# A small addition moved from ScalarE to VectorE, and GpSimd's work per pair of heads in another order

## The chip, the core and the metric

The kernel runs on one core of a Trainium2 chip. TensorE (PE, whose weight loads are listed as PEld), VectorE (DVE), ScalarE (ACT), GpSimd (POOL) and SyncE (SP) each take their own queue of instructions in order. They meet only at semaphores that the program sets and waits for. The metric is the device time of the whole program in microseconds, lower is better. Before the change it is 1112.01 us, the median of 3 runs (1111.71 to 1112.99).

## What is computed

The program chains three parts: attention with rotary position embedding, a mixture of experts, and a dense layer. Only the attention part is touched. Cut to what matters:

```python
def rotate(x):
    x1, x2 = (x[..., :half], x[..., half:])
    return np.concatenate([x1 * cos - x2 * sin, x1 * sin + x2 * cos], axis=-1)
q_rot, k_rot = (rotate(q), rotate(k))          # q, k, v: 4 x 8 heads, 576 positions, 64 wide
scores = scale * np.matmul(q_rot, k_rot.transpose(0, 1, 3, 2))
scores = scores - np.max(scores, axis=-1, keepdims=True)
attn = np.exp(scores)
attn = attn / (np.sum(attn, axis=-1, keepdims=True) + 1e-09)
x = np.matmul(attn, v)                         # then the experts, then the dense layer
```

The `+ 1e-09` on the row sums is the small addition of the title.

## The kernel before

Attention works on 16 pairs of heads. A pair has 9 tiles of scores (`TILES`), numbered 0 to 8: four of 128 rows for head A, one mixed tile with the last 64 rows of both heads (`MIX`, number 4), four for head B. What feeds a product is kept in two halves: a value rounded to fp32r (`hi`) and what is left of it (`lo`).

**PE** runs one `body` per pair, p. In each of its 9 steps it makes a tile of scores of pair p+1 (L376, or L381 and L385 for the mixed tile), turns a tile of probabilities of pair p by transposes against the identity (L423, L419 for the mixed tile, L415 for its corner), and multiplies turned tiles with v (L444, L447, L450). The turned tiles are called A0, X, A1, A2, C, A3, M, B0 to B3. Step 5 turns M (the mixed rows) and multiplies A3. Step 6 makes scores, turns B0, and multiplies M: this product, `MA`, begins with L444, and its first instruction waits until the `lo` half of M is there. The last product of a pair, `MB`, comes in step 1 of the next body.

**ACT** takes the exponential of each tile (L520), rounds each turned tile to `pt_hi` (L541, L535 for X, L538 for C), and moves the sums out of PSUM (L559, L560). In step 3 its `guard` (L551) adds 1e-9, held in a tile `tiny` of one column, to the 9 row sums of pair p: `guarded`.

**DVE** takes the negated maximum of each tile (L620), and `pt_lo` as what `pt_hi` left (L636). In step 5, between the maximum of tile 5 and `pt_lo` of M, `invert` takes the reciprocal of `guarded` (L641). `normalise` (L652, L654, L660) uses it in the next body.

**POOL** prepares pairs ahead. For pair k, `multiply` forms `by_cos` (L338) and `by_sin` (L339) from `raw`. `add_up` forms `rotated` (L323), `hi` (L326) and `lo` (L332). `split_v` splits v of an earlier pair (L312, L317). The order in the loop is multiply(k), split_v(k-2), add_up(k). `split_v(k)` waits for v to have landed, and until PE has done product MB of pair k-2, since it writes over that pair's tile. `add_up(k)` waits for the transfers that read the last `hi`, and its L332 until the scores of pair k-2 are made.

**SP** issues the transfers. Its `body(p)` waits for L332 of pair p+2, and issues 12 copies of `hi` and `lo` into `k_hh`, `k_ll` and `q_st` (the stacks that the scores read). Then it waits for `split_v(p+1)`, loads v of pair p+2 (5 transfers), stores a tail, waits for `multiply(p+3)` and loads `raw` of pair p+4.

Of the kernel before, what the change touches and what calls it, by code (L numbers as in the profile page):

```python
# [11 lines left out]
ALU = mybir.AluOpType  # L12
ACT = mybir.ActivationFunctionType
AX = mybir.AxisListType

P = 128
# [26 lines left out]
def attention(nc, qk, v, cos, sin, ident, fold, emb_t, route_consts, x_all, lg_all, tail_dram,  # L43
# [7 lines left out]
    with ExitStack() as ctx:  # L51
        def sb(name, shape, dt=F32):
            return ctx.enter_context(nc.sbuf_tensor(name, shape, dt))

        def sem(name):
            return ctx.enter_context(nc.semaphore(name))
# [3 lines left out]
        TILES = 2 * FULL + 1  # L60
# [26 lines left out]
        neg_max = [sb(f"neg_max{r}", [P, TILES]) for r in range(2)]  # L87
        row_sum = [sb(f"row_sum{r}", [P, TILES]) for r in range(2)]
        guarded = sb("guarded", [P, TILES])
        tiny = sb("tiny", [P, 1])  # L90
        inv_sum = [sb(f"inv_sum{r}", [P, TILES]) for r in range(2)]
        probs = [sb(f"probs{r}", [P, FULL, 2 * S]) for r in range(2)]
        probs_mix = [sb(f"probs_mix{r}", [P, S]) for r in range(2)]
# [28 lines left out]
        zero_set = sem("zero_set")  # L122
# [14 lines left out]
        exp_done = sem("exp_done")  # L137
# [3 lines left out]
        pv_done = sem("pv_done")  # L141
        o_evac = sem("o_evac")
        fold_ready = sem("fold_ready")
        guard_done = sem("guard_done")
        norm_step = sem("norm_step")
        x_done = sem("x_done")
        tail_stored = [sem(f"tail_stored{r}") for r in range(2)]
# [16 lines left out]
        def _(sp):  # L164
# [43 lines left out]
            def body(p, r, more_raw=True, more=True, first=False, clears=False):  # L208
                if more:

                    sp.wait_ge(rope_done, p + 3)
                    stack_k(r)
                    stack_q(r)

                    sp.wait_ge(v_done, p + 2)
                    load_v(p + 2)
                if not first:
                    store_tail(p - 1, 1 - r)
                if more_raw:

                    sp.wait_ge(mult_done, p + 4)
                    load_raw(p + 4, raw[:], raw_in)
                if clears:
                    for i in range(2):
                        clear(sorted_dram, p * 2 - 2 + i)
# [28 lines left out]

            body(0, 0, first=True)

            sp.wait_ge(zero_set, 2)
            body(1, 1, clears=True)
            with sp.Fori(1, PAIRS // 2 - 2) as m:
                for r in range(2):  # L260
# [35 lines left out]
        @block.gpsimd  # L296
        def _(pool):
            nc.gpsimd.memset(one[:], 1.0)
            nc.gpsimd.memset(raw_v[:, MIX:MIX + 2, :], 0.0)
            nc.gpsimd.memset(raw_v[:, TILES + 1, :], 0.0)  # L300
            for r in range(2):
                nc.gpsimd.memset(q_st[r][0][:, S:WIDE].bitcast(F32), 0.0)
                last = nc.gpsimd.memset(q_st[r][1][:, 0:TAIL].bitcast(F32), 0.0)
            last.then_inc(cleared, 1)

            def split_v(k, r, first=False):

                pool.wait_ge(v_in, (k + 1) * V_LOADS)
                if not first:

                    pool.wait_ge(pv_done, (k - 1) * VALUES)
                nc.gpsimd.tensor_tensor(v_split[r][:, :, 0:DH], raw_v[:],  # L312
                                        one[:].unsqueeze(2).to_broadcast([P, TILES + 2, DH]),
                                        ALU.mult).then_inc(v_hi_done, 1)

                pool.wait_ge(v_hi_done, k + 1)
                nc.gpsimd.tensor_tensor(v_split[r][:, :, DH:2 * DH], raw_v[:], v_split[r][:, :, 0:DH].bitcast(F32),  # L317
                                        ALU.subtract).then_inc(v_done, 1)

            def add_up(k, stacked, count, first=False):  # L320

                pool.wait_ge(mult_done, k + 1)
                nc.gpsimd.tensor_tensor(rotated[:], by_cos[:], by_sin[:], ALU.add)  # L323

                pool.wait_ge(stack_in[stacked], count * STACKS)
                nc.gpsimd.tensor_tensor(hi[:], by_cos[:], by_sin[:], ALU.add).then_inc(hi_rope, 1)  # L326

                if not first:

                    pool.wait_ge(scores_ready, (k - 1) * TILES)  # L330
                pool.wait_ge(hi_rope, k)
                nc.gpsimd.tensor_tensor(lo[:], rotated[:], hi[:].bitcast(F32), ALU.subtract).then_inc(rope_done, 1)  # L332

            def multiply(k):

                pool.wait_ge(raw_in, (k - 1) * 16)
                pool.wait_ge(rope_done, k)
                nc.gpsimd.tensor_tensor(by_cos[:], raw[:, 0:2, :], cos_sb[:], ALU.mult)  # L338
                nc.gpsimd.tensor_tensor(by_sin[:], raw[:, 2:4, :], sin_sb[:], ALU.mult).then_inc(mult_done, 1)  # L339

            pool.wait_ge(cleared, 1)
            add_up(1, 0, 1, first=True)
            multiply(2)
            split_v(0, 0, first=True)
            add_up(2, 1, 1)
            multiply(3)
            split_v(1, 1, first=True)
            add_up(3, 0, 2)
            with pool.Fori(1, PAIRS // 2 - 1) as m:
                multiply(m * 2 + 2)  # L350
                split_v(m * 2, 0)
                add_up(m * 2 + 2, 1, m + 1)
                multiply(m * 2 + 3)
                split_v(m * 2 + 1, 1)
                add_up(m * 2 + 3, 0, m + 2)
            for k in (PAIRS - 2, PAIRS - 1):
                split_v(k, k % 2)

# [155 lines left out]
        def _(act):  # L514
# [27 lines left out]
                                              ACT.Identity)  # L542
                op.then_inc(hi_done, 1)

            def guard(p, r, first=False):

                act.wait_ge(exp_done, (p + 1) * TILES)
                if not first:

                    act.wait_ge(norm_step, p)  # L550
                nc.scalar.activation(guarded[:], row_sum[r][:], ACT.Identity, bias=tiny[:]).then_inc(guard_done, 1)  # L551

            def evac(p, u, first=False):

                act.wait_ge(pv_done, p * VALUES + VALUE["MB" if u else "MA"] + 1)
# [7 lines left out]
            def body(p, r, first=False, second=False, last=False):  # L563
                for i in range(TILES):
                    round_hi(p, r, STEPS[i][0], first)
                    if i == 1 and not first:
                        evac(p - 1, 1, second)
                    if i == 3:
                        guard(p, r, first)
                    if i == 6:  # L570
                        evac(p, 0, first)
                    if not last:
                        exp(p + 1, 1 - r, i)
                    for name in STEPS[i][1:]:
                        round_hi(p, r, name, first)
# [7 lines left out]
                    act.dma_start(fold_sb[u * DH:(u + 1) * DH, :, w * FW:w * FW + E],  # L583
                                  emb_t.rearrange("(g w d) e -> w d g e", w=2, d=DH)[w]).then_inc(consts_in, 16)

            act.wait_ge(zero_set, 2)
            act.wait_ge(tables_in, 32)
            for table in (cos_sb, sin_sb):
                nc.scalar.activation(table[:, 0, :], table[:, 1, :], ACT.Copy, scale=SCALE).then_inc(table_scaled, 1)
# [12 lines left out]
        def _(dve):  # L602
# [34 lines left out]

            def invert(p, r):

                dve.wait_ge(guard_done, p + 1)  # L640
                nc.vector.reciprocal(inv_sum[r][:], guarded[:]).then_inc(norm_step, 1)  # L641

            def normalise(p, r, u, stores=None):

                dve.wait_ge(norm_step, p + 1)

                dve.wait_ge(fold_ready, p * 2 + u + 1)
                at = u * (MIX + 1)
# [25 lines left out]
                    if i == 3 and not first:  # L674
                        normalise(p - 1, 1 - r, 1, stores)

            nc.vector.memset(tiny[:], 1e-9).then_inc(zero_set, 1)
            nc.vector.memset(zeros[:], 0.0).then_inc(zero_set, 1)
            dve.wait_ge(tables_in, 32)
            rope_first(1, first_k_in, first_k_mult, first_k_done)  # L680

# [1042 lines left out]
```

## Time and profile before

| | us |
|---|---|
| median of 3 runs | 1112.01 |
| profiled execution, its own time | 1112.01 |
| its span | 1110.2 |
| PE busy | 986.5 (89%) |
| DVE busy | 595.4 (54%) |
| ACT busy | 581.9 (52%) |
| POOL busy | 414.9 (37%) |

All rows further down are of this one execution. The span runs from the first recorded instruction to the last. The time of the execution is 1.81 us more. A row of a timeline gives the start in us from the span's start, the duration in us, the engine and line, the operation with what it writes and reads, how many instructions are merged in it, and in brackets how long the engine was idle before it and what ended that. Attention fills the span from its start to about 348 us.

### The profile page before, as it was taken

The numbers are of one execution on the slowest core, as the hardware profiler recorded it, in microseconds if no ns is written. First come the engines' busy times: TensorE is split into PE (matmuls) and PEld (weight loads), VectorE is DVE, ScalarE is ACT, GpSimd is POOL, SyncE is SP. The second block draws the span as 40 slices with busy tenths as digits, with TensorE's granted clock in tenths as the row PEclk, the third lists the DMA queues.
The fourth block names the chain that finished last, engine by engine and source line by source line (L and its number), as shares of the span: only waits on it lengthen the run. The fifth ranks groups of instructions, "written<-read, shape, count | busy, mean of one in ns | idle before, by whom it ended". The sixth has DMA issues, their size and how long they took to land. (4 is left out here: it accounts for less than half of the span.)

```text
span 1110.2 us, 18954 instructions
## 1 busy us (share of the span) xinstructions
PE 986.5 (89%) x5604; PEld 871.3 (78%) x5605; DVE 595.4 (54%) x1195; ACT 581.9 (52%) x1273; POOL 414.9 (37%) x246
## 2 busy tenths in 40 slices
PE   1999999999995039999999975999999999999996
PEld 1899998988984038888888865888989989899895
DVE  4677777777773721111111103777666666666764
ACT  1677777777772632222222214666565565655653
POOL 3988878788610429309948305000000000000000
PEclk9999999999998559999999997999999999999999
DMA  8777686776713455314433106211000000000001
GB/s 236 192 206 183 182 213 166 209 193 170 192 62 90 161 191 199 104 41 146 163 123 113 38 29 195 64 48 48 1 15 14 0 28 0 11 17 0 28 2 28
DMA packets 63078, 113.82 MB, mean 103 GB/s; under 512 B 20033, under 2 KB 24641, under 8 KB 61121
## 3 DMA queue, kind: packets, MB, share of 16 engines
q1 hardware_dynamic: 52352, 92.62, 29.4%
q10 hardware_dynamic: 7808, 11.31, 3.1%
q0 software_dynamic: 2880, 9.44, 2.5%
q8 instruction: 18, 0.29, 0.1%
q14 instruction: 20, 0.16, 0.0%
HBM read 60.58 MB, written 24.41 MB: 77 GB/s over the span
## 5 line engine op out<-in xcount | busy, mean ns | idle before, releaser
L1432 PE MATMUL hd_ps<-y_hi,w_hi 128*128 128x384 f32 x384 | 131.1, 341 | 7.7 <-DVE g_sb L1602 6.9
L1432 PE MATMUL hd_ps<-y_lo,w_hi 128*128 128x384 f32 x384 | 129.4, 337 | 0.0
L1432 PE MATMUL hd_ps<-y_hi,w_lo 128*128 128x384 f32 x384 | 129.1, 336 | 0.0
L1502 ACT ACTIVATE mag<-hd_ps 128x384 f32<-128x384 f32 x96 | 47.3, 493 | 151.7 <-PE hd_ps L1432 149.2
L620 DVE TENSOR_REDUCE neg_max<-ps 128x1 f32<-128x576 f32 x144 | 108.1, 750 | 32.7 <-PE ps L376 30.2
L636 DVE TENSOR_TENSOR pt_lo<-ps,pt_hi 128x512 fp32r<-128x512 f32 x144 | 99.2, 690 | 43.5 <-ACT pt_hi L541 41.8
L541 ACT ACTIVATE pt_hi<-ps 128x512 fp32r<-128x512 f32 x144 | 86.8, 603 | 60.8 <-PE ps L423 59.5
L1450 PE MATMUL o_ps<-w_hi,g_hi 128*128 128x512 f32 x288 | 114.8, 399 | 2.2 <-DVE g_lo L1611 2.2
L1450 PE MATMUL o_ps<-w_hi,g_lo 128*128 128x512 f32 x288 | 114.1, 396 | 0.0
L1450 PE MATMUL o_ps<-w_lo,g_hi 128*128 128x512 f32 x288 | 113.3, 393 | 0.0
L1611 DVE TENSOR_TENSOR g_lo<-g_sb,g_hi 128x384 fp32r<-128x384 f32 x96 | 53.6, 558 | 111.2 <-ACT g_hi L1517 111.2
L520 ACT ACTIVATE probs<-ps,neg_max 128x576 f32<-128x576 f32 x128 | 95.4, 745 | 25.7 <-DVE neg_max L620 25.4
L423 PE MATMUL ps<-id_sb,probs 128*128 128x128 f32 x576 | 87.8, 279 | 5.4 <-DVE pt_lo L636 5.1
L1105 POOL TENSOR_TENSOR w_hi<-w_stage,one 128x1024 f32 (+1 forms) x32 | 60.6, 1895 | 80.4 <-ACT h_row L1208 61.7
L447 PE MATMUL ps<-pt_hi,v_split 128*128 128x256 f32 (+1 forms) x320 | 85.8, 350 | 1.9 <-issue 0.5
L1432 PEld LDWEIGHTS hd_ps<-y_hi,w_hi 128*128 128x128 f32 x384 | 72.5, 189 | 17.0 <-DVE g_sb L1602 13.9
L376 PE MATMUL ps<-k_hh,q_st 128*128 128x288 f32 x256 | 59.4, 315 | 24.9 <-DMA q_st<-qk_lo 22.9
L1278 DVE TENSOR_TENSOR h_lo<-ht_ps,h_hi 128x512 fp32r<-128x512 f32 x40 | 25.8, 686 | 98.3 <-ACT h_hi L1233 98.3
L1109 POOL TENSOR_TENSOR w_lo<-w_stage,w_hi 128x1024 f32 (+1 forms) x32 | 76.7, 2396 | 4.6 <-POOL w_hi L1105 4.0
L423 PEld LDWEIGHTS ps<-id_sb,probs 128*128 128x128 f32 x576 | 67.7, 142 | 11.2 <-DVE pt_lo L636 9.4
L1432 PEld LDWEIGHTS hd_ps<-y_lo,w_hi 128*128 128x128 f32 x384 | 72.4, 189 | 3.0
L1271 DVE TENSOR_TENSOR x_lo<-xt_ps,x_hi 128x512 fp32r<-128x512 f32 x20 | 13.8, 692 | 111.7 <-ACT x_hi L1216 111.7
(208 smaller groups left out, 2431.6 us busy)
## 6 DMA issues: line engine op xcount, KB each, us to landing
w_stage<-in_w SPq DMA_DIRECT2D x32, 512.0 KB, 3.6
raw_qk<-in_qk SPq DMA_DIRECT2D x14, 1152.0 KB, 6.5
k_hh<-qk_hi SPq DMA_DIRECT2D x64, 144.0 KB, 5.0
k_ll<-qk_lo SPq DMA_DIRECT2D x64, 144.0 KB, 5.0
sorted_rows<-zeros SPq DMA_DIRECT2D x28, 256.0 KB, 6.5
x_row<-sorted_rows ACTq DMA_DIRECT2D x20, 256.0 KB, 2.7
y_rows<-y_row ACTq DMA_DIRECT2D x20, 256.0 KB, 2.1
q_st<-qk_hi SPq DMA_DIRECT2D x32, 144.0 KB, 4.5
```

What stands on the lines that cost most here:

```text
L376: last = nc.tensor.matmul(dst[:, a:z], q_st[r][u][:, at:at + P], keys[r][u][:, key:key + z - a], start=h == 0, stop=h == 1)
L423: last = nc.tensor.transpose(dst[:, j * P:(j + 1) * P], probs[r][:, j, key:key + P], id_sb[:])
L447: nc.tensor.matmul(ps[:, CUT - MAIN // 2 - P + a:CUT - MAIN // 2 - P + z], main, pt_hi[:, k, a:z], start=begin, stop=False)
L520: nc.scalar.activation(dst, score[(r + i) % 2], ACT.Exp, bias=neg_max[r][:, i:i + 1], accum_out=row_sum[r][:, i:i + 1]).then_inc(exp_done, 1)
L541: op = nc.scalar.activation(pt_hi[:, FULL if name == "M" else int(name[1]), P:P + MAIN], src, ACT.Identity)
L620: nc.vector.tensor_reduce(neg_max[r][:, i:i + 1], score[(r + i) % 2], AX.X, ALU.max, negate=True).then_inc(max_done, 1)
L636: nc.vector.tensor_tensor(lo_at, src, hi_at.bitcast(F32), ALU.subtract).then_inc(lo_done, 1)
L1105: nc.gpsimd.tensor_tensor(chunk_of(w_hi, slot, c), stage[:, c % RING, :], one[:].to_broadcast([P, CHUNK]), ALU.mult).then_inc(w_hi_done, 1)
L1109: nc.gpsimd.tensor_tensor(chunk_of(w_lo, slot, c), stage[:, c % RING, :], chunk_of(w_hi, slot, c).bitcast(F32), ALU.subtract).then_inc(w_s ...
L1432: op = nc.tensor.matmul(hd_ps[f % 2][:, 0:G], w[:, c, cols], y[:, c, :], start=c == 0 and h == 0, stop=c == DC - 1 and h == 2)
L1450: op = nc.tensor.matmul(o_ps[:, i, :], a[f % 2][:, rows], w[:, f, :], start=f == 0 and h == 0, stop=f == KF - 1 and h == 2)
L1611: nc.vector.tensor_tensor(g_lo[f % 2][:], g_sb[f % 2][:], g_hi[f % 2][:].bitcast(F32), ALU.subtract).then_inc(glo_done, 1)
```

## The change

It has three parts.

1. ACT no longer adds 1e-9. `invert` on DVE does it, with a tensor_tensor of `row_sum` and `tiny` into `guarded`, right ahead of the reciprocal. `tiny` now has 9 columns. The reciprocal waits for this addition through the semaphore `norm_step`, which now counts two per pair, and `guard_done` is gone.
2. On POOL `multiply` and `add_up` of a pair are one function, `rope`, and stand together. `split_v(k-2)` comes ahead of both, not between them.
3. Of the two memsets at the start on DVE only the second raises `zero_set`. ACT does not wait for it any more, DVE itself and SP do.

```diff
-        tiny = sb("tiny", [P, 1])
+        tiny = sb("tiny", [P, TILES])
-            sp.wait_ge(zero_set, 2)
+            sp.wait_ge(zero_set, 1)
-            def multiply(k):
+            def rope(k, stacked, count):
                 pool.wait_ge(raw_in, (k - 1) * 16)
                 pool.wait_ge(rope_done, k)
                 nc.gpsimd.tensor_tensor(by_cos[:], raw[:, 0:2, :], cos_sb[:], ALU.mult)
                 nc.gpsimd.tensor_tensor(by_sin[:], raw[:, 2:4, :], sin_sb[:], ALU.mult).then_inc(mult_done, 1)
+                add_up(k, stacked, count)
...
             with pool.Fori(1, PAIRS // 2 - 1) as m:
-                multiply(m * 2 + 2)
                 split_v(m * 2, 0)
-                add_up(m * 2 + 2, 1, m + 1)
-                multiply(m * 2 + 3)
+                rope(m * 2 + 2, 1, m + 1)
                 split_v(m * 2 + 1, 1)
-                add_up(m * 2 + 3, 0, m + 2)
+                rope(m * 2 + 3, 0, m + 2)
...
-            def guard(p, r, first=False):
-                act.wait_ge(exp_done, (p + 1) * TILES)
-                if not first:
-                    act.wait_ge(norm_step, p)
-                nc.scalar.activation(guarded[:], row_sum[r][:], ACT.Identity, bias=tiny[:]).then_inc(guard_done, 1)
...
-            act.wait_ge(zero_set, 2)
...
             def invert(p, r):
-                dve.wait_ge(guard_done, p + 1)
+                dve.wait_ge(exp_done, (p + 1) * TILES)
+                nc.vector.tensor_tensor(guarded[:], row_sum[r][:], tiny[:], ALU.add).then_inc(norm_step, 1)
+                dve.wait_ge(norm_step, p * 2 + 1)
                 nc.vector.reciprocal(inv_sum[r][:], guarded[:]).then_inc(norm_step, 1)
             def normalise(p, r, u, stores=None):
-                dve.wait_ge(norm_step, p + 1)
+                dve.wait_ge(norm_step, p * 2 + 2)
...
-            nc.vector.memset(tiny[:], 1e-9).then_inc(zero_set, 1)
+            nc.vector.memset(tiny[:], 1e-9)
             nc.vector.memset(zeros[:], 0.0).then_inc(zero_set, 1)
+            dve.wait_ge(zero_set, 1)
```

In step 5 of a body, DVE's queue held these rows before (`neg_max` is the maximum of a tile, `pt_lo` the low half of a turned one; the second `pt_lo` is that of M):

```order
L636 TENSOR_TENSOR pt_lo<-ps,pt_hi 128x512
L620 TENSOR_REDUCE neg_max<-ps 128x1
L641 RECIPROCAL inv_sum<-guarded 128x9
L636 TENSOR_TENSOR pt_lo<-ps,pt_hi 128x512
L620 TENSOR_REDUCE neg_max<-ps 128x1
```

and it holds these now, with the lines of the changed kernel:

```order
L621 TENSOR_TENSOR pt_lo<-ps,pt_hi 128x512
L605 TENSOR_REDUCE neg_max<-ps 128x1
L626 TENSOR_TENSOR guarded<-row_sum,tiny 128x9
L628 RECIPROCAL inv_sum<-guarded 128x9
L621 TENSOR_TENSOR pt_lo<-ps,pt_hi 128x512
L605 TENSOR_REDUCE neg_max<-ps 128x1
```

One instruction was put in ahead of the low half of M. Both of its inputs lie in SBUF.

On POOL, one pass of the loop over a pair was this before:

```order
L338 TENSOR_TENSOR by_cos<-raw_qk,cos_sb 128x1152
L339 TENSOR_TENSOR by_sin<-raw_qk,sin_sb 128x1152
L308 REGISTER_ALU
L311 REGISTER_ALU
L312 TENSOR_TENSOR v_split<-raw_v,one_a 128x11x64
L317 TENSOR_TENSOR v_split<-raw_v,v_split 128x11x64
L322 REGISTER_ALU
L323 TENSOR_TENSOR rotated<-by_cos,by_sin 128x1152
L325 ISA
L326 TENSOR_TENSOR qk_hi<-by_cos,by_sin 128x1152
```

and is this now:

```order
L310 REGISTER_ALU
L311 TENSOR_TENSOR v_split<-raw_v,one_a 128x11x64
L316 TENSOR_TENSOR v_split<-raw_v,v_split 128x11x64
L335 REGISTER_ALU
L337 TENSOR_TENSOR by_cos<-raw_qk,cos_sb 128x1152
L338 TENSOR_TENSOR by_sin<-raw_qk,sin_sb 128x1152
L321 REGISTER_ALU
L322 TENSOR_TENSOR rotated<-by_cos,by_sin 128x1152
L324 ISA
L325 TENSOR_TENSOR qk_hi<-by_cos,by_sin 128x1152
L329 REGISTER_ALU
L331 TENSOR_TENSOR qk_lo<-rotated,qk_hi 128x1152
```

The two instructions of `split_v` moved ahead of the two products. What follows them kept its place.

## Rows read from the trace of the kernel before

**Rows 1.** Busy time by stretch: from:to, length, PE, PEld, DVE, ACT, POOL, PEclk, DMA, GB/s.

```profile
60.00:240.00 180.00, 174.64 (x1340) 163.81 (x1340) 133.26 (x243) 131.58 (x316) 145.91 (x64) 1.00 0.73 189
```

**Rows 2.** Waits from 40 to 345 us: who waited, us in total, times, longest.

```profile
POOL by_cos L338 <- DMA raw_qk<-in_qk: 40.1, 12, 4.0
```

**Rows 3.** The page's DMA issues: count, KB each, median us to landing.

```profile
raw_qk<-in_qk SPq DMA_DIRECT2D x14, 1152.0 KB, 6.5
```

**Rows 4.** Timeline of SP in one pair (pair 6 on PE).

```profile
164.25 1.24 SPq L193 DMA_DIRECT2D q_st<-qk_lo  x2
169.79 0.36 SPq L173 DMA_DIRECT2D raw_v<-in_v  x1
...
174.61 0.37 SPq L167 DMA_DIRECT2D raw_qk<-in_qk  x1
```

**Rows 5.** Timeline of POOL over one pass of its loop.

```profile
140.84 2.65 POOL L338 TENSOR_TENSOR by_cos<-raw_qk,cos_sb 128x1152 f32<-128x1152 f32 x1 [3.72 <-DMA raw_qk<-in_qk]
...
146.07 1.36 POOL L312 TENSOR_TENSOR v_split<-raw_v,one_a 128x704 fp32r<-128x704 f32 x1
147.51 1.70 POOL L317 TENSOR_TENSOR v_split<-raw_v,v_split 128x704 fp32r<-128x704 f32 x1
149.17 2.65 POOL L323 TENSOR_TENSOR rotated<-by_cos,by_sin 128x1152 f32<-128x1152 f32 x1
151.76 2.67 POOL L326 TENSOR_TENSOR qk_hi<-by_cos,by_sin 128x1152 fp32r<-128x1152 f32 x1
154.58 2.67 POOL L332 TENSOR_TENSOR qk_lo<-rotated,qk_hi 128x1152 fp32r<-128x1152 f32 x1
```

**Rows 6.** Timeline of PE, first scores of pair 12.

```profile
250.41 0.52 PE L376 MATMUL ps<-k_hh,q_st 128*128 128x288 f32 x2 [0.58 <-DMA q_st<-qk_lo]
```

**Rows 7.** Timeline of DVE, the reciprocals of pairs 10, 11 and 13.

```profile
242.11 0.20 DVE L641 RECIPROCAL inv_sum<-guarded 128x9 f32<-128x9 f32 x1
...
262.26 0.20 DVE L641 RECIPROCAL inv_sum<-guarded 128x9 f32<-128x9 f32 x1
...
301.88 0.20 DVE L641 RECIPROCAL inv_sum<-guarded 128x9 f32<-128x9 f32 x1
```

**Rows 8.** Timeline of DVE around the reciprocal of pair 6.

```profile
163.95 0.75 DVE L620 TENSOR_REDUCE neg_max<-ps 128x1 f32<-128x576 f32 x1
164.61 0.20 DVE L641 RECIPROCAL inv_sum<-guarded 128x9 f32<-128x9 f32 x1
164.85 0.69 DVE L636 TENSOR_TENSOR pt_lo<-ps,pt_hi 128x512 fp32r<-128x512 f32 x1
...
166.52 0.69 DVE L636 TENSOR_TENSOR pt_lo<-ps,pt_hi 128x512 fp32r<-128x512 f32 x1 [0.31 <-ACT pt_hi L541]
```

**Rows 9.** Timeline of PE's weight loads there: turning B0, then product MA.

```profile
165.12 0.50 PEld L423 LDWEIGHTS ps<-id_sb,probs 128*128 128x128 f32 x4
165.59 0.19 PEld L444 LDWEIGHTS ps<-pt_hi,v_split 128*128 128x128 f32 x1
```

**Rows 10.** Timeline of ACT around the addition of pair 6, to M.

```profile
159.37 0.29 ACT L551 ACTIVATE guarded<-row_sum,tiny 128x9 f32<-128x9 f32 x1
...
162.71 0.60 ACT L541 ACTIVATE pt_hi<-ps 128x512 fp32r<-128x512 f32 x1 [1.37 <-PE ps L423]
...
164.22 0.60 ACT L541 ACTIVATE pt_hi<-ps 128x512 fp32r<-128x512 f32 x1 [0.19 <-PE ps L423]
```

**Rows 11.** Timeline of DVE in the routing part: small instructions that wait for one another.

```profile
361.48 0.17 DVE L891 TENSOR_TENSOR emb_n<-emb_n 128x8 f32<-128x8 f32 x1
361.68 0.17 DVE L892 TENSOR_TENSOR emb_n<-emb_n 128x8 f32<-128x8 f32 x1
```

**Rows 12.** Timeline of DVE in `normalise`: small instructions with no wait between them.

```profile
173.59 0.18 DVE L652 TENSOR_TENSOR router_shares<-ps,inv_sum 128x32 f32 x1
173.71 0.42 DVE L654 TENSOR_TENSOR token_rows<-ps,inv_sum 128x256 f32 x1
```

**Rows 13.** Timeline of PE: the end of product MB of pair 5.

```profile
155.55 0.40 PE L450 MATMUL ps<-pt_lo,v_split 128*128 128x256 f32 x2
```

More of the change, by code:

```diff
@@ L143, in attention @@
         fold_ready = sem("fold_ready")
-        guard_done = sem("guard_done")
         norm_step = sem("norm_step")
@@ L339, in multiply @@
                 nc.gpsimd.tensor_tensor(by_sin[:], raw[:, 2:4, :], sin_sb[:], ALU.mult).then_inc(mult_done, 1)
+                add_up(k, stacked, count)
             pool.wait_ge(cleared, 1)
             add_up(1, 0, 1, first=True)
-            multiply(2)
             split_v(0, 0, first=True)
-            add_up(2, 1, 1)
-            multiply(3)
+            rope(2, 1, 1)
             split_v(1, 1, first=True)
-            add_up(3, 0, 2)
+            rope(3, 0, 2)
             with pool.Fori(1, PAIRS // 2 - 1) as m:
-                multiply(m * 2 + 2)
                 split_v(m * 2, 0)
-                add_up(m * 2 + 2, 1, m + 1)
-                multiply(m * 2 + 3)
+                rope(m * 2 + 2, 1, m + 1)
                 split_v(m * 2 + 1, 1)
-                add_up(m * 2 + 3, 0, m + 2)
+                rope(m * 2 + 3, 0, m + 2)
             for k in (PAIRS - 2, PAIRS - 1):
@@ L567, in body @@
                         evac(p - 1, 1, second)
-                    if i == 3:
-                        guard(p, r, first)
                     if i == 6:
```

## The prediction

> **What bounds the kernel now.** I first read where PE's time goes by stretch, since PE has the most busy time. In the attention part PE is busy for 174.64 of 180 us, at the full clock (PEclk 1.00) [rows 1], so whatever keeps PE waiting there costs time one for one. A pair takes 19.38 us: the reciprocal of pair 6 starts at 164.61 and that of pair 10 at 242.11, 77.50 us for four pairs [rows 7, 8].
>
> Then I read the waits. POOL waits 40.1 us in 12 waits for the load of `raw` [rows 2]. That tells that POOL and SP run in a ring with its own period. One turn: L332 of a pair ends at 154.58 + 2.67 = 157.25 [rows 5]. SP then issues the 12 copies, the last at 164.25 for 1.24, to 165.49. It sits still until 169.79, since `split_v` of the same pass has yet to end, then issues v, the tail and, at 174.61, `raw` [rows 4]. This lands 6.5 us later [rows 3], near 181.1. So `raw` lands 23.9 us after L332 ended, and from it POOL has all its seven instructions to go. In the steady state L332 ends one turn after the last, and the load that it waits for was issued a turn earlier: period T = 23.9 - T + work. Work from the start of L338 to the end of L332 is 157.25 - 140.84 = 16.41 [rows 5], so T = 40.3 / 2 = 20.2 us. The ring is slower than PE by 0.8 us a pair, and overtakes its lead at pair 12: PE waits 0.58 us for `q_st` there [rows 6]. The three periods from pair 10 to pair 13 take 301.88 - 242.11 = 59.77 us [rows 7], against 3 x 19.38 = 58.14. So the ring costs 1.6 us in the whole program.
>
> Last I read, in the order of time, what stands around L551 and L641.
>
> **The change part by part.** *POOL's order.* `split_v` now needs no `raw`, and can run as soon as L332 of the pair before has ended. It takes 149.17 - 146.07 = 3.10 us [rows 5], so it is over 3.1 us after L332, well before SP is through with its 12 copies (8.2 us). SP's wait of 169.79 - 165.49 = 4.3 us goes. `raw` is issued 4.82 us after 165.49 instead of 169.79 [rows 4], 13.1 us after L332, and lands at 19.6. Now POOL's turn is split_v (3.1), then the products and `add_up`, 13.3. With `raw` there, T = 19.6 - T + 13.3 gives 16.5, and POOL's own work also gives 16.4. Both are below 19.38, so PE leads the ring and the late waits go: -1.6 us. What is late next is `split_v` itself, which waits until PE has done MB. It has a turn less 16.4, some 3 us, to spare. In the first three pairs nothing changes, since there POOL works without a break and the same instructions come before each `add_up`.
>
> *ACT.* The 16 instructions L551 of 0.29 us go. After each, ACT idles 1.37 us until PE has turned A3, and 0.19 us for M [rows 10]. What it saves ends in these: 0 us. If instead the exponential of that step were what PE waits for, 0.2 us a pair would be gained; there are idle 1.37 us in between, so I take 0.
>
> *DVE.* Here the change adds to the path. `pt_lo` of M starts at 164.85 [rows 8], 0.03 us after ACT's rounding of M ends (164.22 + 0.60) [rows 10], and ends at 165.54. PE's load for L444 starts at 165.59 [rows 9]. PE comes there itself at this time: 0.47 us after the first load of the four transposes before it. So DVE has no slack in front of MA. It is the only thing queued that matters: behind the new addition wait the reciprocal, `pt_lo` of M, then the next maximum and `pt_lo` of B0, which has 0.31 us to spare [rows 8].
>
> The addition would start where the reciprocal now does, at 164.61. The reciprocal follows 0.20 us later, the spacing of two small instructions of which the second waits for the first [rows 11]. From it to `pt_lo` of M are 0.12 us at least (spacing of a 0.18 us instruction and one that doesn't wait for it [rows 12]) and 0.24 at most (now, L641 to L636 [rows 8]). So `pt_lo` starts 0.32 to 0.44 us after 164.61, not 0.24: 0.08 to 0.20 later. I take 0.13, nearer to the row without a wait, since `pt_lo` does not wait for the reciprocal. PE waits as much before L444. ACT's move of the sums waits for MA and the last turns of the pair for ACT, so nothing of it is regained. In 15 pairs (the last has no maxima on DVE, and slack): 15 x 0.13 = +2.0 us. The bounds are 1.2 and 3.0, and 0 if an unseen slack in PE of 0.1 us hides it.
>
> *The start.* ACT's wait for the memsets had long been met, and `tiny` of 9 columns costs nothing: 0.
>
> **Sum.** 1112.01 - 1.6 + 2.0 = 1112.4 us. The profiled execution took 1112.01 us, and its span 1110.2, so 1.81 us lie around it. It is also the median.
>
> **The rivals.** *A, the addition has to wait for POOL's instruction beside it (slower).* All that DVE does next to a tensor instruction of POOL in this trace has at most one input in SBUF, the other in PSUM. The new addition has two in SBUF. No row shows such a pair of instructions overlap, so the cost of one is open from 0 to a whole instruction of POOL, 2.65 us [rows 5]. What decides is which of them comes first. In the new order POOL's `split_v` starts when MB is done. MB of pair 5 ends at 155.55 + 0.40 = 155.95 [rows 13]. With a wake-up of 0.15 (as L326's end to L332's start [rows 5]) `split_v` starts at 156.10. `by_cos` follows 3.10 later at 159.20, `rotated` 5.23 (146.07 - 140.84 [rows 5]) and a wake-up of 0.2 later at 164.6. The addition is due at 164.61: the same moment. If POOL is first, the addition starts when `rotated` ends, 2.6 us late, and PE loses 2.6 us. From pair 2 to pair 12, in which POOL runs with this phase, that is 11 x 2.6 = 28.6 us. In pairs 0 and 1 the addition falls in the last 0.5 us of a product of POOL, 1 us for both. The sum would be 1112.4 + 29.6 = 1142. Since the phase differs by about 0.1 us between even and odd pairs, it can also hit half of them: about 1128. If the addition comes first it costs only the 1 us of the first pairs: 1113.4. It decides from the first pair in which POOL wins. For it speaks that the two are due together, against it that the addition is queued behind a running instruction of DVE and needs no wake-up, while `rotated` needs one.
>
> The Trainium skill states a rule for this, in "SBUF — State Buffer", section "SBUF: two separate sides": VectorE and GpSimd share a pair of ports, a VectorE instruction with two SBUF inputs contends for it with a GpSimd instruction that reads SBUF, and whichever starts first holds it for its whole instruction while the other is fully blocked. No run here shows it yet. By this rule A's prices would hold, and without it the addition would be free of POOL: that moves my chance of A up from what the rows alone would give (they are silent), and changes no number of the sum.
>
> *B, the addition is hidden (faster).* If PE has an unseen slack before L444, only the ring's 1.6 us go: 1110.4. Against it speaks that L444 follows the end of `pt_lo` by 0.05 us.
>
> *C, POOL's order gives nothing.* If SP is held by something else than `split_v`, the ring keeps 20.2 us. Then PE has waits at pairs 12 to 14 as before, which swallow what DVE adds to the pairs up to 11, and only 3 x 0.13 = 0.4 us remain: 1112.4. For it speaks only that SP's queue is full, against it the gap of 4.3 us in SP's rows. The time doesn't tell C from the forecast, the waits do.
>
> **How the numbers follow.** Forecast 0.50. Its own range is 1111.6 to 1114.4: 15 x 0.08 to 15 x 0.20 less the 1.6, and at the upper end the 1 us of the first two pairs, if POOL wins only there. A with losses in half or in all of the pairs 0.33, in equal parts. B 0.08, C 0.09. A measurement of this kernel can tell a change of about 0.2%, 2.2 us. The forecast, B and C lie within it, 0.67 together; B has 1.6 of the 2.2 us, so I give 0.06 of these to faster by over 0.2%, a B with something regained on top, and 0.61 stay for the same. Slower is A, 0.33. The range goes from B, 1110.3, to half of A, 1130, and leaves out the full A (0.16) and a little below.
>
> **What would show it.** POOL's wait for `raw` (40.1 us) is gone, and in its place `split_v` L312's match waits for PE L450 in every pair. SP no longer waits for `split_v`. PE's waits for `q_st` at pairs 12 to 14 are gone. A wait of 0.1 to 0.2 us before the load of L444's match in 15 pairs would show my DVE step right; one of 2.6 us in even or in all pairs, with `pt_lo` of M that much later, would show A. The forecast is wrong if the period of a pair in the middle is more than 0.25 us from 19.38, or if the late waits stay.

## The result

The changed kernel takes 1142.25 us, the median of 4 runs (1141.73 to 1142.58), against 1112.27 us for the kernel before in the same session (4 runs, 1111.71 to 1112.99). The ratio is 1.0269 [1.0251, 1.0287]: slower by 30.0 us. The forecast of 1112.4 and its range, up to 1130, were wrong. Rival A, in its full form, had 1142, with a chance of 0.16, and the range left it out.

The page of the profiled execution (1142.72 us, its span 1140.9) gives the busy time of each engine:

```profile
span 1140.9 us, 18958 instructions
PE 993.9 (87%) x5604; PEld 881.5 (77%) x5605; DVE 624.4 (55%) x1211; ACT 580.4 (51%) x1257; POOL 415.8 (36%) x246
```

The same stretch as in [rows 1] (length, then PE, PEld, DVE, ACT, POOL busy, PEclk, DMA share, GB/s). PE had 174.64 us there, and the full clock:

```profile
60.00:240.00 180.00, 161.33 (x1191) 152.13 (x1190) 136.39 (x222) 117.15 (x275) 135.37 (x60) 0.96 0.67 179
```

The waits from 40 to 375 us (total, times, longest), to set beside [rows 2]. POOL's wait for `raw` is gone, `split_v` waits for MB instead, and no wait of PE for `q_st` is left from 230 us on. That is what the POOL step said. But PE now waits for `pt_lo` of M before MA's first load (L440), 28.2 us in 14 waits, where the forecast had 15 waits of 0.1 to 0.2:

```profile
POOL v_split L311 <- PE ps L446: 53.9, 13, 16.3
...
PEld ps L440 <- DVE pt_lo L621: 28.2, 14, 2.5
```

The addition itself, all sixteen of it in one row (shortest, median, longest in ns; start of the first and the last):

```profile
L626 DVE TENSOR_TENSOR guarded<-row_sum,tiny x16: 158/2524/2611, 48.5 to 366.7; 128x9 f32<-128x9 f32 x16
```

The median, 2.52 us, is nearly the length of one of POOL's big instructions (2.64), and the shortest lasts 0.16 us. The time line of pair 6, POOL and DVE, to be compared with [rows 5, 8]:

```profile
173.59 2.67 POOL L338 TENSOR_TENSOR by_sin<-raw_qk,sin_sb 128x1152 f32<-128x1152 f32 x1
176.34 2.64 POOL L322 TENSOR_TENSOR rotated<-by_cos,by_sin 128x1152 f32<-128x1152 f32 x1
178.94 2.64 POOL L325 TENSOR_TENSOR qk_hi<-by_cos,by_sin 128x1152 fp32r<-128x1152 f32 x1
...
176.47 2.53 DVE L626 TENSOR_TENSOR guarded<-row_sum,tiny 128x9 f32<-128x9 f32 x1
179.04 0.21 DVE L628 RECIPROCAL inv_sum<-guarded 128x9 f32<-128x9 f32 x1
179.17 0.66 DVE L621 TENSOR_TENSOR pt_lo<-ps,pt_hi 128x512 fp32r<-128x512 f32 x1
```

`rotated` starts 0.13 us ahead of the addition and ends at 178.98. The addition ends at 179.00, 0.02 us later. DVE counts as busy for all that time, so no table of waits names POOL: the stall stands in the instruction's own length. In what follows such an addition is called held, by the POOL instruction beside it. `pt_lo` of M follows, and only then PE, which had come to the end of its four turns (the transposes of B0) at 177.72:

```profile
177.12 0.60 PE L419 MATMUL ps<-id_sb,probs 128*128 128x128 f32 x4
179.88 0.33 PE L440 MATMUL ps<-pt_hi,v_split 128*128 128x128 f32 x1 [2.17 <-DVE pt_lo L621]
180.57 0.57 PE L372 MATMUL ps<-k_hh,q_st 128*128 128x288 f32 x2
180.94 0.68 PE L372 MATMUL ps<-k_ll,q_st 128*128 128x288 f32 x2
...
184.37 0.43 PE L372 MATMUL ps<-k_ll,q_st 128*128 128x288 f32 x2
```

The additions of pairs 2 to 12 last 2.52 to 2.61 us, those of pairs 0 and 1 0.48 and 0.79, and those of pairs 13 to 15, beside which no instruction of POOL runs, 0.16. Pair 13 shows the free form, with the reciprocal 0.19 and `pt_lo` of M 0.32 us behind the addition's start:

```profile
331.60 0.16 DVE L626 TENSOR_TENSOR guarded<-row_sum,tiny 128x9 f32<-128x9 f32 x1
331.79 0.21 DVE L628 RECIPROCAL inv_sum<-guarded 128x9 f32<-128x9 f32 x1
331.92 0.66 DVE L621 TENSOR_TENSOR pt_lo<-ps,pt_hi 128x512 fp32r<-128x512 f32 x1
```

The last rows look at the clock. PE's rows above are slower from 180.57 to about 184 (0.68 us for what takes 0.43 at 184.37). Six times, after the wait in every second pair from pair 2 to pair 12, the granted clock is at its lower level of 1.2 GHz for about 3.4 us. Otherwise it is at 2.4 GHz from 41 us to the end of the attention part. Before and after the fall in pair 6, then two whole pairs, one without a fall and one with:

```profile
176.00:180.00 4.00, 1.83 (x14) 1.59 (x14) 3.96 (x5) 1.95 (x4) 3.92 (x3) 1.00 0.61 162
180.60:184.00 3.40, 3.40 (x18) 3.38 (x17) 1.94 (x3) 2.98 (x8) 0.98 (x1) 0.52 0.77 271
...
201.40:223.60 22.20, 19.01 (x144) 17.70 (x144) 17.15 (x30) 14.18 (x33) 16.50 (x8) 1.00 0.67 185
223.60:245.70 22.10, 20.09 (x144) 19.22 (x144) 16.70 (x27) 14.12 (x33) 15.90 (x8) 0.92 0.58 158
```

Before the fall of pair 6 the engine had waited 2.17 us, until 0.7 us before its slower rows begin. The odd pairs have such a wait too (2.23 us in pair 7), and no fall.

### The profile page after: what moved, and what is told of

Read it like the earlier page. It is cut to its first block and busy times, and to the rows that moved or that the text cites. A ratio compares the mean times of both kernels' runs of the same rounds, so it can differ in the third digit from the quotient of the medians.

```text
span 1140.9 us, 18958 instructions
## 1 busy us (share of the span) xinstructions
PE 993.9 (87%) x5604; PEld 881.5 (77%) x5605; DVE 624.4 (55%) x1211; ACT 580.4 (51%) x1257; POOL 415.8 (36%) x246
## 3 DMA queue, kind: packets, MB, share of 16 engines
q1 hardware_dynamic: 52352, 92.62, 28.2%
## 5 line engine op out<-in xcount | busy, mean ns | idle before, releaser
L419 PE MATMUL ps<-id_sb,probs 128*128 128x128 f32 x576 | 91.1, 289 | 4.0 <-DVE pt_lo L621 3.7
L419 PEld LDWEIGHTS ps<-id_sb,probs 128*128 128x128 f32 x576 | 72.6, 148 | 7.2 <-DVE pt_lo L621 6.2
```

What stands on the lines that cost most here:

```text
L419: last = nc.tensor.transpose(dst[:, j * P:(j + 1) * P], probs[r][:, j, key:key + P], id_sb[:])
```

## The experiments

The kernels were measured in several sessions, each with the kernel before on the same chip. In two of these (e5, e6, e7 and e9; e10 and e11) the kernel before itself ran from 1110.6 to 1122.1 us, and the traces taken there are longer behind the attention part: 763.8 to 771.5 us from its end to the end of the span, against 761.5 to 762.7 in the other six traces. So beside each ratio stands the length of the attention part in the profiled execution, from PE's first product to the end of the last instruction that writes `tail_sb`. The order alone, traced in two sessions, has 325.22 and 325.30 us, so this length repeats to 0.1. It is 327.04 us for the kernel before, which was traced once, and 356.70 for the changed one: 29.66 more, of the 30.7 by which the two profiled executions differ. For the changed kernel and for e1 to e4 the ratio and the attention part agree to about 0.6 us. In the two later sessions the ratio gives 1.0 to 2.9 us more than the attention part does, which lies outside attention and is not explained. These rows give the ends, for before, changed, and the order alone:

```profile
348.18 0.23 DVE L660 TENSOR_TENSOR tail_sb<-ps,inv_sum 128x80 f32<-128x80 f32 x1
```

```profile
378.01 0.23 DVE L647 TENSOR_TENSOR tail_sb<-ps,inv_sum 128x80 f32<-128x80 f32 x1
```

```profile
346.45 0.23 DVE L657 TENSOR_TENSOR tail_sb<-ps,inv_sum 128x80 f32<-128x80 f32 x1
```

| kernel | ratio to before | attention, us | addition, pairs 2 to 12 |
|---|---|---|---|
| changed | 1.0269 [1.0251, 1.0287] | 356.70 | 2.52 to 2.61 |
| e1, order only | 0.9986 [0.9975, 0.9996] | 325.22 | on ACT |
| e11, the same | 0.9996 [0.9981, 1.0010] | 325.30 | on ACT |
| e2, addition only | 1.0047 [1.0032, 1.0063] | 332.40 | 0.16 to 1.02 |
| e3, one SBUF input | 1.0259 [1.0231, 1.0287] | 356.07 | 2.52 to 2.61 |
| e4, small memsets | 1.0261 [1.0235, 1.0287] | 355.48 | 2.54 to 2.62 |
| e9, wide memsets | 1.0029 [1.0012, 1.0045] | 327.42 | 0.16 |
| e5, later on DVE | 1.0022 [1.0001, 1.0043] | 327.00 | 0.94 to 1.02 |
| e10, earlier on DVE | 1.0049 [1.0027, 1.0072] | 331.13 | 0.45 to 0.56 |
| e6, no addition | 0.9997 [0.9980, 1.0013] | 325.68 | none |
| e7, as a reduction | 1.0008 [0.9992, 1.0024] | 326.23 | 0.16 |

**e1 and e2: the two parts apart.** e1 is the kernel before with POOL's part of the change and nothing else. The addition stays on ACT:

```diff
-            def multiply(k):
+            def rope(k, stacked, count):
...
+                add_up(k, stacked, count)
...
-                multiply(m * 2 + 2)
...
-                add_up(m * 2 + 2, 1, m + 1)
+                rope(m * 2 + 2, 1, m + 1)
```

> The kernel before with POOL's new order alone; the 1e-9 is still added on ACT. Theory P (the new addition on DVE waits until the POOL instruction that runs beside it has ended): no such addition here, so no loss, and POOL's ring falls from 20.2 us to PE's period, so the late waits of PE for q_st (pairs 12 to 14) go: 1110.7 us, 1.6 below before. Rival O (the new order of POOL is what costs, since split_v now waits for PE): about 1142 us, as after.

Measured: 1111.65 us (10 runs) against 1113.28. Repeated:

> The kernel before with POOL's new order alone, once more with more rounds: 1.6 us less than before by the late waits of PE for q_st, ratio 0.9985 (0.9975 to 0.9995). The rival is that the first measured ratio was chance, and the order gives nothing: 1.000.

Measured: 1116.60 us (12 runs) against 1117.47 (18 runs). The reciprocals of pairs 10 to 13 lie 19.36, 19.41 and 19.34 us apart, where those of [rows 7] took 59.77 for the three:

```profile
242.04 0.20 DVE L638 RECIPROCAL inv_sum<-guarded 128x9 f32<-128x9 f32 x1
...
300.15 0.20 DVE L638 RECIPROCAL inv_sum<-guarded 128x9 f32<-128x9 f32 x1
```

The late waits are gone, and the attention part is 1.8 and 1.7 us shorter in the two traces. The times only half bear it out: one interval lies below 1, the other holds it. e1 also answers a question of the addition: its reciprocal has one input in SBUF, starts behind POOL's `rotated` just as the addition does, and is not held:

```profile
164.38 2.67 POOL L323 TENSOR_TENSOR rotated<-by_cos,by_sin 128x1152 f32<-128x1152 f32 x1
...
164.54 0.20 DVE L638 RECIPROCAL inv_sum<-guarded 128x9 f32<-128x9 f32 x1
```

e2 is the changed kernel with POOL's old order:

```diff
-                rope(m * 2 + 2, 1, m + 1)
+                multiply(m * 2 + 2)
...
+                add_up(m * 2 + 2, 1, m + 1)
```

> The changed kernel with POOL's old order (multiply, split_v, add_up); the addition is on DVE. P: the addition meets other POOL instructions at other moments, and lasts between 0.16 and 2.6 us instead of always 2.5; where a DVE delay is 1 us on average over 13 pairs, 1112 + 13 = 1125 us, bounds 1115 and 1142. Rival O: 1112 to 1114 us. Rival W (what costs is the addition's wait and its hand-over to the reciprocal, whatever POOL does): 1142 us as after, with the addition 2.5 us long in every pair.

Measured: 1119.23 us (7 runs) against 1113.28, less than the 1125 expected and inside its bounds. The attention part is 5.4 us longer than before. In the old order POOL starts when `raw` has landed, so its phase to DVE shifts from pair to pair, and the addition is held for anything from 0 to 1.17 us, from pair 1 on by the second instruction of `split_v`. Pair 9:

```profile
226.93 1.70 POOL L316 TENSOR_TENSOR v_split<-raw_v,v_split 128x704 fp32r<-128x704 f32 x1
227.64 1.01 DVE L629 TENSOR_TENSOR guarded<-row_sum,tiny 128x9 f32<-128x9 f32 x1
228.59 2.65 POOL L322 TENSOR_TENSOR rotated<-by_cos,by_sin 128x1152 f32<-128x1152 f32 x1
228.69 0.21 DVE L631 RECIPROCAL inv_sum<-guarded 128x9 f32<-128x9 f32 x1
```

The addition ends 0.02 us after the instruction that it met, although POOL's next one, which reads SBUF too, follows that one at once: the waiting DVE instruction goes ahead of POOL's next. In none of the traces is an addition held for longer than what is left of one POOL instruction. Nor does its own 0.16 us come on top. In pair 4 `v_split` has 0.10 us left, and the addition lasts no longer than a free one:

```profile
126.77 1.69 POOL L316 TENSOR_TENSOR v_split<-raw_v,v_split 128x704 fp32r<-128x704 f32 x1
...
128.36 0.16 DVE L629 TENSOR_TENSOR guarded<-row_sum,tiny 128x9 f32<-128x9 f32 x1
128.42 2.67 POOL L322 TENSOR_TENSOR rotated<-by_cos,by_sin 128x1152 f32<-128x1152 f32 x1
```

The two parts do not add: the order alone gives -1.8 us, the addition alone +5.4, both +29.7. The new order ties POOL's start to MB's end, and so puts the start of `rotated` just ahead of the addition in every pair from 2 to 12, by 0.13 us in the even pairs and 0.06 in the odd ones.

**e3: one input instead of two.** Is it the second SBUF input that makes the addition wait?

```diff
-                nc.vector.tensor_tensor(guarded[:], row_sum[r][:], tiny[:], ALU.add).then_inc(norm_step, 1)
+                nc.vector.tensor_scalar(guarded[:], row_sum[r][:], 1e-9, None, ALU.add).then_inc(norm_step, 1)
```

> The changed kernel, but the addition is a tensor_scalar with 1e-9 as an immediate: one input in SBUF, same place, same waits. P in the form that counts inputs: the instruction lasts 0.17 us in all pairs, L440's wait shrinks to 0.1 us: 1112 to 1113 us. A form of P in which any small fp32 instruction between SBUF and SBUF can be held up: 2.5 us in 11 pairs, 1142 us. Rival W: 1142 us as well. Rival O: 1142 us.

Measured: 1142.69 us (4 runs). No gain. Pairs 1 and 2:

```profile
69.81 2.66 POOL L322 TENSOR_TENSOR rotated<-by_cos,by_sin 128x1152 f32<-128x1152 f32 x1
...
69.78 0.16 DVE L626 TENSOR_SCALAR guarded<-row_sum 128x9 f32<-128x9 f32 x1
...
88.95 2.63 POOL L322 TENSOR_TENSOR rotated<-by_cos,by_sin 128x1152 f32<-128x1152 f32 x1
...
89.09 2.52 DVE L626 TENSOR_SCALAR guarded<-row_sum 128x9 f32<-128x9 f32 x1
```

Here the race itself is seen. In pair 1 DVE starts 0.03 us before `rotated` and takes 0.16 us. In pair 2 it starts 0.14 us after and takes 2.52. In pair 3 the lead of `rotated` is 0.06 us (110.76 and 110.82), and the addition takes 2.60. The number of SBUF inputs is not what decides: this addition has one and is held, the reciprocal has one and is free. The Trainium skill gives `tensor_scalar` a mode that reads one SBUF tensor through both ports ("VectorE: DVE Perf Modes", section "Mode 2×_2P — use both read ports for one tensor"), and says that such a form contends with GpSimd and `tensor_reduce` never does ("SBUF — State Buffer", section "Who interferes with whom"). This run agrees for the first, with 2.52 us for 0.16, and the next one for the second.

**e7: the same sum as a reduction.** `row_sum` gets a second column that always holds 1e-9, and the addition becomes a reduction over the two:

```diff
-        row_sum = [sb(f"row_sum{r}", [P, TILES]) for r in range(2)]
+        row_sum = [sb(f"row_sum{r}", [P, TILES, 2]) for r in range(2)]
...
-                                     accum_out=row_sum[r][:, i:i + 1]).then_inc(exp_done, 1)
+                                     accum_out=row_sum[r][:, i:i + 1, 0]).then_inc(exp_done, 1)
...
-                nc.vector.tensor_tensor(guarded[:], row_sum[r][:], tiny[:], ALU.add).then_inc(norm_step, 1)
+                nc.vector.tensor_reduce(guarded[:], row_sum[r][:], AX.X, ALU.add).then_inc(norm_step, 1)
...
-            nc.vector.memset(tiny[:], 1e-9)
+            for r in range(2):
+                nc.vector.memset(row_sum[r][:, :, 1], 1e-9)
```

> The changed kernel; the addition at the same place of DVE and with the same waits, but as a tensor_reduce over two columns, row_sum and a constant 1e-9 side by side in one tile: one input in SBUF. The tensor_scalar with one input was held up, so the number of inputs alone does not decide. Theory P2 (held up are the forms that read SBUF through both of DVE's ports, which a tensor_tensor with two SBUF inputs and a tensor_scalar do, and a reduction or reciprocal does not): 0.17 us in all pairs beside rotated, 1112.4 us, ratio to before 1.000 (0.999 to 1.002). If every instruction of DVE that waits for nothing and starts beside a fresh POOL instruction were held: 1142 us.

Measured: 1118.28 us (12 runs) against 1117.46 (33 runs). All sixteen are free, also where `rotated` has started first:

```profile
L625 DVE TENSOR_REDUCE guarded<-row_sum x16: 162/164/165, 48.0 to 335.7; 128x9 f32<-128x18 f32 x16
...
164.28 2.68 POOL L321 TENSOR_TENSOR rotated<-by_cos,by_sin 128x1152 f32<-128x1152 f32 x1
...
164.43 0.16 DVE L625 TENSOR_REDUCE guarded<-row_sum 128x9 f32<-128x18 f32 x1
```

This is the clearest of the runs. The addition stays on DVE, at its place, with POOL's new order and twice the columns, and the whole loss is gone. So it is not DVE's queue, nor the place, but the form of the instruction beside POOL's.

**e4 and e9: move `rotated` behind the addition.** Both put memsets on POOL between `by_sin` and `add_up`, which delays `rotated`. They write SBUF and read nothing. e4:

```diff
+                for i in range(4):
+                    nc.gpsimd.memset(spare[:, i:i + 1], 0.0)
                 add_up(k, stacked, count)
```

> The changed kernel, with four memsets of one column on POOL ahead of rotated, so that rotated starts some 0.2 to 0.4 us later in every pair and the addition on DVE comes first. P with 'who starts first holds': the addition lasts 0.16 us in pairs 2 to 12, rotated is held back by at most 0.2 us, and the time falls to 1112 to 1114 us. If instead POOL always wins, or an overlap of any order slows the addition: stays 1142 us. Rivals W and O: 1142 us.

Measured: 1141.99 us (4 runs). A miss: the memsets took 0.23 us for the four, and POOL's two instructions lie as close together as without them. `rotated` still starts 0.08 us after the end of `by_sin` (173.81 + 2.68), and still ahead of the addition, at 176.70:

```profile
176.40 0.23 POOL L341 MEMSET spare<- 128x1 f32 x4
176.57 2.65 POOL L323 TENSOR_TENSOR rotated<-by_cos,by_sin 128x1152 f32<-128x1152 f32 x1
```

So this run does not test the other order of the starts in pairs 2 to 12. Only in pair 1 does the addition lead, by 0.08 us (68.96 and 69.04), and there it takes 0.16.

e9 makes them wide enough, three of 256 columns:

```diff
+                for i in range(3):
+                    nc.gpsimd.memset(spare[:, i, :], 0.0)
                 add_up(k, stacked, count)
```

> The changed kernel with three memsets of 256 columns on POOL ahead of rotated; the four small ones before had moved rotated by 0.03 us only. These should take some 0.9 us, so that rotated starts 0.6 to 0.9 us after the addition is due, in all pairs. P with 'who starts first holds': the addition lasts 0.16 us in pairs 2 to 12 (memsets read nothing), and the time is 1112 to 1113 us. If POOL wins at any order: 1142 us. If memsets hold the addition too: it lasts up to 0.9 us, about 1120 us.

Measured: 1121.19 us (10 runs) against 1117.46, attention 0.4 us longer than before. From pair 2 on every addition takes 0.16 us, here while a memset runs:

```profile
166.99 0.81 POOL L341 MEMSET spare<- 128x256 f32 x3
...
167.27 0.16 DVE L629 TENSOR_TENSOR guarded<-row_sum,tiny 128x9 f32<-128x9 f32 x1
...
167.77 2.65 POOL L323 TENSOR_TENSOR rotated<-by_cos,by_sin 128x1152 f32<-128x1152 f32 x1
```

Against the changed kernel only the memsets are new. They put `rotated` behind the addition, POOL has more work, and yet 29.3 us of attention go. That shows the order of the two starts as the cause. It shows too that a POOL instruction which only writes does not hold the addition. The 1121.19 us are above the 1112 to 1113 expected. The kernel before, measured together with e9, was 5 us slower than in the first runs as well. Of the rest, 0.4 lies in the attention part, and some 3 us outside it.

**e5 and e10: move the addition.** e5 calls `invert` at the end of DVE's part of a pair, e10 ahead of the maximum of step 5 instead of behind it:

```diff
-                    if i == 5:
-                        invert(p, r)
...
+                invert(p, r)
```

> The changed kernel with the addition and the reciprocal at the end of the body on DVE, behind the low half of B3, instead of in step 5. There DVE idles over 1 us before the next maximum. The addition still has two SBUF inputs and falls into the last 1 us of POOL's qk_lo. Theory P (held until the POOL instruction beside it ends, whichever started first): it lasts up to 1 us in pairs 2 to 12, but that fits into DVE's idle time, and nothing is added in step 5: 1110.7 us, as the kernel before with POOL's new order alone (ratio to before 0.998 to 0.999). If the wait for POOL cost time wherever it is: at least 1120 us.

```diff
+                    if i == 5:
+                        invert(p, r)
                     maximum(p, r, i)
```

> The changed kernel with the addition and reciprocal one place earlier on DVE, ahead of the maximum of tile 5. They are due 0.66 us earlier, while POOL's by_sin has some 0.5 us left to run. Theory P (an instruction that comes second waits for the rest of the one that runs, and then goes ahead of the next one, as in pair 1): the addition lasts about 0.6 us in pairs 2 to 12 instead of 2.5, the low half of M comes about 0.4 us late, and the time is 1115 to 1118 us. If POOL's next instruction goes ahead of a waiting addition: it lasts 3 us or more, and the time is above 1145 us. If the 2.5 us are a price of the addition at any place beside POOL: 1142 us.

Measured: 1119.54 us (12 runs) against 1117.46, and 1122.90 us (5 runs) against 1117.47. In both most of the 30 us is gone, and in neither is the addition free in pairs 0 to 12. From pair 1 on it meets another POOL instruction that has 0.4 to 1.1 us left, `qk_lo` in e5 and `by_sin` in e10, and is held for the rest of it:

```profile
170.37 2.65 POOL L331 TENSOR_TENSOR qk_lo<-rotated,qk_hi 128x1152 fp32r<-128x1152 f32 x1
...
172.12 0.93 DVE L626 TENSOR_TENSOR guarded<-row_sum,tiny 128x9 f32<-128x9 f32 x1
```

```profile
185.35 2.66 POOL L338 TENSOR_TENSOR by_sin<-raw_qk,sin_sb 128x1152 f32<-128x1152 f32 x1
...
187.47 0.56 DVE L626 TENSOR_TENSOR guarded<-row_sum,tiny 128x9 f32<-128x9 f32 x1
188.08 2.65 POOL L322 TENSOR_TENSOR rotated<-by_cos,by_sin 128x1152 f32<-128x1152 f32 x1
```

In both each addition is longer by about what is left of POOL's instruction. For e10 the sixteen additions last 5.4 us more than 16 x 0.16, and the attention part is 5.9 us longer than that of e1. For e5 they last 11.2 us more in sum, but the attention part is only 1.8 us longer than that of e1. The expectation had named idle time of DVE at that place, which would take up the rest. e5 was expected to cost nothing against e1, so it missed by these 1.8 us. e10 was expected at 3 to 6 us over the kernel before and came out at 5.4, its attention part at 4.1.

**e6: no addition at all**, to see what ACT's had cost. The reciprocal reads `row_sum`, and the 1e-9 is left out of the computation:

```diff
-                nc.vector.tensor_tensor(guarded[:], row_sum[r][:], tiny[:], ALU.add).then_inc(norm_step, 1)
-                dve.wait_ge(norm_step, p * 2 + 1)
-                nc.vector.reciprocal(inv_sum[r][:], guarded[:]).then_inc(norm_step, 1)
+                nc.vector.reciprocal(inv_sum[r][:], row_sum[r][:]).then_inc(norm_step, 1)
```

> The changed kernel without the addition of 1e-9 on any engine: the reciprocal on DVE reads row_sum itself (this leaves the 1e-9 out of the computation). If ACT's addition cost nothing, as I predicted, this equals the kernel before with POOL's new order alone: ratio to before 0.9985. If ACT's 16 x 0.29 us lay on the path: 4.6 us less, ratio 0.9945. P and O differ here as well: by O (the order alone costs) it would be 1142 us.

Measured: 1116.94 us (12 runs) against 1117.46. Its attention part is 325.68 us, against 325.22 and 325.30 with the addition on ACT. So no cost of the sixteen additions on ACT is to be seen, where their 16 x 0.29 = 4.6 us would have been.

## Why the prediction was wrong

The step that failed is the DVE term, "15 x 0.13 = +2.0". It priced the addition by its free length alone and put the wait for POOL at nothing, and left the other case, in which the addition waits for `rotated`, to rival A. In its place the runs showed a wait of 2.36 or 2.44 us in each of 11 pairs, 26.4 us in all.

Which of the two cases holds hung on one comparison, "`rotated` at 164.6" against "the addition is due at 164.61". The prediction called it the same moment and then chose the side on which DVE comes first. (Its own terms, 155.95 + 0.15 + 3.10 + 5.23 + 0.2, give 164.63, so `rotated` 0.02 us behind the addition.) The measured phases decide for the other side, by a little:

```profile
167.41 0.40 PE L446 MATMUL ps<-pt_lo,v_split 128*128 128x256 f32 x2
167.89 1.36 POOL L311 TENSOR_TENSOR v_split<-raw_v,one_a 128x704 fp32r<-128x704 f32 x1 [3.81 <-PE ps L446]
```

Starting from MB's end at 167.81, `split_v` starts 0.08 us later, where 0.15 was taken. From it to `rotated` are 176.34 - 167.89 = 8.45 us, where 3.10 + 5.23 + 0.2 = 8.53 was taken. Together that is 0.15 us sooner. From MB's end to the addition are 8.66 us, as forecast, so `rotated` leads by 0.13 us instead of trailing by 0.02. The argument "needs no wake-up" for DVE weighed too little, since POOL's own wake-up is only 0.08 us, from the end of MB's last instruction to `split_v` as from the end of `by_sin` to `rotated` (176.26 to 176.34). With an outcome of 2 us on one side and 30 on the other, and a comparison good to 0.1 us at best, the chances of 0.50 and 0.33 rested on nothing in the trace.

The other steps, one by one:
- POOL's order: right. The waits for `raw` and for `q_st` go, and -1.6 us were forecast, -1.8 and -1.7 seen in the traces (e1, e11).
- ACT: right, 0 (e6). The start: PE's first product comes at 21.54 us, and the others lie between 21.0 and 23.3 with either start, so no cost is to be seen.
- The free part of the DVE term: the reciprocal 0.19 and `pt_lo` 0.32 us after the addition (pair 13), 0.08 us later than before and so at the low bound. A late pair without a wait (13 to 14) takes 19.47 us, 0.07 over the same one in e1, which makes 1.0 us in 15 pairs, and e7 as a whole is 1.0 us longer than e1. So 1.0 us, not 2.0.
- Rival A: right in mechanism, in place and in its pairs: 11 held by `rotated`, two that meet the end of a product, three free. Its sum is right to 0.3 us, but that is luck: errors cancel in it. It priced a held addition at 2.6 us, 28.6 in all. It is 2.36 us over the free 0.16 in the even pairs and 2.44 in the odd ones, in all 26.4 us for pairs 2 to 12, and 0.95 for pairs 0 and 1. The free part was 1.0 too high. And it had no term for the clock. From the reciprocal of an odd pair to that of the next even one e7 takes 19.50 us and the changed kernel, with no fall, 21.86, which is the 2.36 and no more. From an even pair to the next odd one e7 takes 19.40 us and the changed kernel, with a fall, 22.40, which is the 2.44 and another 0.56. In e4 four of the five falls come in odd pairs, and the period from an odd pair to the next even one is 22.40 to 22.44 with a fall and 21.87 without: 0.54. In e3, compared in the same way, a fall costs 0.56 to 0.76. For the changed kernel I take 0.55 us a fall, and 3.3 for the six.

The account against e1, whose attention is 31.5 us shorter: 26.4 + 0.95 + 3.3 + 1.0 gives 31.7.

The clock's part was not separated by an experiment of its own. What the traces show is that all the falls belong to kernels with waits of 2.5 us: six in the changed kernel, five in e3, five in e4, and none in the other nine traces from 45 us to the end of the attention part. In e3 they do not come in every second pair (they follow pairs 4, 6, 8, 9 and 12), and the longer periods between reciprocals (22.42 to 22.57 us, against 21.81 to 21.87 for the others between pairs 2 and 12) go with them and not with the number of the pair. Why only some of the equal waits are followed by a fall stays open.

What also stays open is how near a tie can be: a lead of 0.06 us for POOL held the addition, and DVE's lead of 0.03 (e3) left it free. The runs show which forms are held, by what and for how long. That it is ports which the two engines share, none of them shows by itself. Of the waits in pairs 0 and 1, which vary from run to run (0.16 to 1.44 us), only the sizes were read.

## What to carry to other kernels

Before a small instruction goes to DVE in the critical chain, look at what POOL runs in that moment, and whether both read SBUF in a form that excludes the other: it can then cost the rest of POOL's instruction, here 2.4 us for 0.16 us of work. Two starts within 0.1 us of each other are not a forecast but a coin, and a change of order that ties the two engines to one event throws it once for all pairs. The cure is cheap once it is seen: the same work in a form that does not contend (a reduction here), or left on an engine with idle time. Of all versions only the one with POOL's new order and the addition left on ACT has ever had its whole interval below that of no change (0.9986), and its repetition could not tell it from no change.

## What the runs showed of the hardware that was not expected

- A held DVE instruction shows as a long one, not as idle time: 2.52 to 2.61 us for 0.16 us of work, ending 0.02 to 0.04 us after POOL's instruction, and it goes ahead of POOL's next one (e2). With 0.10 us of POOL's instruction left it lasts 0.16 us, as a free one does.
- `tensor_scalar` on one SBUF tensor of 9 fp32 columns is held like the addition of two (e3), the reciprocal (e1) and a reduction (e7) are not, and a POOL memset holds nothing (e9).
- After waits of 2.2 us in PE, one in each turn of about 22 us, the granted clock fell from 2.4 to 1.2 GHz for about 3.4 us, in the changed kernel 0.6 to 1.2 us after the wait had ended and in every second pair, at about 0.55 us each (e3: up to 0.76).
- Four memsets of one column on POOL took 0.23 us together, and the two dependent POOL instructions around them were still only 0.08 us apart (e4).
